# Queries on the state as four 64x64 tiles in two banks, with two weight pieces split by a summing transfer and the Nyquist row moved behind the mixing

## The reference, cut to what matters

```python
for t in range(S):
    state = alpha[:, :, t, :, None] * state + np.einsum('bhd,bhe->bhde', k[:, :, t], v[:, :, t])
    y[:, :, t] = np.einsum('bhd,bhde->bhe', q[:, :, t], state)
```

## Time and profile before

| | us |
|---|---|
| median of 3 runs | 721.84 |
| lowest, highest | 718.55, 721.86 |
| the profiled execution's own time | 720.12 |
| its span in the profile | 718.3 |

### The profile page before, as it was taken

The page is one execution under the profiler, slowest core; times in us unless marked ns, Lnnn a source line. Parts: engine busy times, 40 slices in busy tenths (PEclk is TensorE's granted clock), DMA queues, the critical chain, the costliest instruction groups (busy, mean ns, idle before and its releaser), DMA issues.

```text
span 718.3 us, 13452 instructions
## 1 busy us (share of the span) xinstructions
PE 701.0 (98%) x5578; PEld 670.6 (93%) x5578; DVE 451.8 (63%) x869; ACT 198.4 (28%) x369; POOL 80.0 (11%) x124
## 2 busy tenths in 40 slices
PE   7799989999999999999999999999999999999998
PEld 6689989889998999989999999999999999999998
DVE  7997868897768977668687747372543817331212
ACT  1438111242113411134415332232211422222111
POOL 1023000030001200042110512002210101000000
PEclk9999999999999999999999999999999999999999
DMA  9757132231332223061324403002110200000000
GB/s 295 208 139 182 52 100 84 83 97 55 91 93 71 63 54 97 35 212 44 112 77 165 144 20 92 1 34 67 53 59 1 76 23 33 0 34 1 5 29 34
DMA packets 21214, 55.90 MB, mean 78 GB/s; under 512 B 2388, under 2 KB 14808, under 8 KB 21160
## 3 DMA queue, kind: packets, MB, share of 16 engines
q1 hardware_dynamic: 18104, 44.53, 20.1%
q0 software_dynamic: 2912, 10.47, 5.6%
q10 hardware_dynamic: 144, 0.13, 0.1%
HBM read 45.66 MB, written 9.46 MB: 77 GB/s over the span
## 4 chain that ended last, share of the span: by engine, by line
PE 86%; DVE 10%; issue 2%; ACT 1%; DMA 1%; DVEq 0%; SPq 0%
PE bank L1178 74%; PE bank L1209 3%; PE bank L1241 2%; PE bank L1236 1%; PE bank L1273 1%; PE bank L1402 1%; PE bank L1388 1%; PE bank L1226 1%; DVE fwd L927 1%; DVE rev L915 1%; PE bank L1199 1%; DVE u_kept L1138 1%; DMA decay_k_q<-in_akq 1%; DVE sm L945 1%; DVE gated L1029 1%
## 5 line engine op out<-in xcount | busy, mean ns | idle before, releaser
L1178 PE MATMUL bank<-ut_hi,w_c 128*128 128x384 f32 x576 | 162.6, 338 | 0.0
L1125 DVE SCALAR_TENSOR_TENSOR hidden_lo<-bank,hidden_hi 128x384 fp32r<-128x384 f32 x96 | 53.3, 556 | 155.5 <-ACT hidden_hi L849 154.9
L1178 PEld LDWEIGHTS bank<-ut_hi,w_c 128*128 128x128 f32 x576 | 105.4, 188 | 0.4
L849 ACT ACTIVATE hidden_hi<-bank 128x384 fp32r<-128x384 f32 x96 | 47.2, 492 | 201.6 <-PE bank L1178 200.5
L1178 PE MATMUL bank<-w_c_hi,hidden_hi 128*128 128x384 f32 x288 | 96.6, 335 | 0.5 <-DVE u_kept L1138 0.5
L1178 PE MATMUL bank<-ut_lo,w_c 128*128 128x384 f32 x288 | 96.3, 334 | 0.0
L1178 PE MATMUL bank<-w_c_hi,hidden_lo 128*128 128x384 f32 x288 | 96.3, 334 | 0.0
L1178 PE MATMUL bank<-w_c_lo,hidden_hi 128*128 128x384 f32 x288 | 96.2, 334 | 0.0
L1178 PE MATMUL bank<-w_sg_hi,vn_hi 128*128 128x384 f32 x192 | 67.1, 350 | 0.0
L1178 PE MATMUL bank<-w_sg_lo,vn_hi 128*128 128x384 f32 x192 | 64.9, 338 | 0.0
L1178 PE MATMUL bank<-w_sg_hi,vn_lo 128*128 128x384 f32 x192 | 64.9, 338 | 0.0
(11 more groups left out here) (193 smaller groups left out, 1339.8 us busy)
## 6 DMA issues: line engine op xcount, KB each, us to landing
decay_k_q<-in_akq SPq DMA_DIRECT2D x19, 673.8 KB, 5.0
x_scratch<-x_half SPq DMA_DIRECT2D x8, 579.0 KB
out_tiles<-u_kept SPq DMA_DIRECT2D x24, 192.0 KB, 2.0
values<-in_v SPq DMA_DIRECT2D x18, 192.0 KB, 5.0
x_quarters<-x_scratch SPq DMA_DIRECT2D x16, 168.9 KB
raw_first_a<-in_w_first SPq DMA_DIRECT2D x3, 768.0 KB, 10.2
raw_first_b<-in_w_first SPq DMA_DIRECT2D x3, 768.0 KB
raw_weights_b<-in_w_second SPq DMA_DIRECT2D x3, 768.0 KB
```

The costliest lines, as they stand in the source:

```text
L849: nc.scalar.activation(hid[0][:, i % 4, :], HB[i % 2][:, 0:HS], ACT.Relu).then_inc(hhi_done, 1)
L1125: nc.vector.scalar_tensor_tensor(out=hid[1][:, i % 4, :], in0=HB[i % 2][:, 0:HS], scalar=0.0, in1=f32(hid[0][:, i % 4, :]), op0=ALU.max, o ...
L1178: ins = nc.tensor.matmul(dst, a, c, start=start and n == 0, stop=stop and n == len(passes) - 1)
```

## The change

In words:

1. **Queries on the state.** In step "out" all matmuls with values now come first, head by head, the first head of each pair to `ky` and the second to `sc[1]`, the bank with the second head's scores. The wait for `std_done` and the queries on the state come behind them, each head by itself: 48 rows, 64 columns of weights, 48 columns moving, in the order group, head, half. `y_done` rises by 4 for each chunk instead of 2, and all its waits are changed to match. ACT's copy gathers from the two banks.
2. **Pieces 6 and 7** of the weights join `SUMMED`. ACT's cast of piece 6 moves behind the four copies of z, that of piece 7 from step s 2 to behind the statistics of s 3; each is followed by the negative, and GpSimd issues the adding transfer there. DVE does nothing for them. The load of pieces 7 and 8 waits for the cast of the piece before instead of its subtraction.
3. **Nyquist** stands behind mix 0 on all engines, writes columns from 388 on of `FB[0]` and `FB[1]`, and waits for nothing of its own; ACT makes two copies instead of one. PE's wait for `ahr_done` goes; ACT waits for `ny_done` ahead of the copies of mix 1 and 2. GpSimd's step nyquist, and with it the gathering transfers of the quarters, moves behind its step mix 0, which waits for DVE's first statistics of that mixing.

The diff, cut to its core:

```diff
-SUMMED = (2, 3, 4)
+SUMMED = (2, 3, 4, 6, 7)
@@ P2_AT (P2_FIRST_AT in the same way)
-         10: [("nyquist", 0), ("mix", 0)], 11: [("stats", 0)],
+         10: [("mix", 0), ("nyquist", 0)], 11: [("stats", 0)],
@@ LAST_P1_AT
-              ("s", 1): [("split", 6), ("z", 0), ("z", 1), ("z", 2), ("z", 3)],
-              ("s", 2): [("nyquist", 0), ("split", 7), ("mix", 0), ("stats", 0)],
-              ("s", 3): [("mix", 1), ("stats", 1)], ("s", 4): [("mix", 2)],
+              ("s", 1): [("z", 0), ("z", 1), ("z", 2), ("z", 3), ("split hi", 6), ("neg", 6)],
+              ("s", 2): [("mix", 0), ("nyquist", 0), ("stats", 0)],
+              ("s", 3): [("mix", 1), ("stats", 1), ("split hi", 7), ("neg", 7)], ("s", 4): [("mix", 2)],
@@ GpSimd, phase1
+                            if what == "neg":
+                                sum_lo(n)
@@ ScalarE
-                nc.scalar.copy(yn[n % 2][:, c, :], ky[:, 0:DM]).then_inc(yn_done, 1)
+                nc.scalar.copy(yn[n % 2][:, c, :].rearrange("p (g j d) -> p j g d", j=2, d=D),
+                               banks[:, at - 1:at + 1, 0:G * D].rearrange("p j (g d) -> p j g d", g=G)[:, ::-1]
+                               ).then_inc(yn_done, 1)
...
-                    nc.scalar.copy(by_channel(fourier_tiles(m)[4][:]), by_parity(FB[1][0:1, 0:NL])).then_inc(ahr_done, 1)
+                    for odd in range(2):
+                        ins = nc.scalar.copy(by_channel(fourier_tiles(m)[4][:])[:, 0, odd], FB[odd][0:1, 2 * NL:2 * NL + KQ])
+                    ins.then_inc(ahr_done, 1)
                 if step == "mix":
                     act.wait_ge(mix_done, 2 * (KD * m + i + 1))
+                    if i > 0:
+                        act.wait_ge(ny_done, m + 1)
@@ TensorE, attend, step "out"
+                    y = [ky, sc[1]]
+                    for g in range(G):
+                        for j in range(2):
+                            cols = slice((2 * g + j) * D, (2 * g + j + 1) * D)
+                            for q in QUERIES:
+                                ins = nc.tensor.matmul(y[j][q, g * D:(g + 1) * D], sm[:, g, j, q], values[:, cols],
+                                                       start=g == 0, stop=c == 0, skip_group_check=True)
+                                if c == 0 and g == G - 1:
+                                    ins.then_inc(y_done, 1)
                     if c >= 1:
                         pe.wait_ge(std_done, (NT - 1) * n + c)
-                    for g in range(G):
-                        if c >= 1:
-                            for q in QUERIES:
-                                nc.tensor.matmul(ky[q, g * PP:(g + 1) * PP], qu[:, g, q], std[:, c % 2, g, :],
-                                                 start=True, stop=False, skip_group_check=True)
-                        ...
+                        for g in range(G):
+                            for j in range(2):
+                                at = slice(j * HR, j * HR + D)
+                                for q in QUERIES:
+                                    ins = nc.tensor.matmul(y[j][q, g * D:(g + 1) * D], qu[at, g, q],
+                                                           std[at, c % 2, g, j * D:(j + 1) * D], start=False, stop=True,
+                                                           skip_group_check=True)
+                                    if g == G - 1:
+                                        ins.then_inc(y_done, 1)
@@ TensorE, mixing and phase 2
-                    pe.wait_ge(z_kept, 4 * m + 2)
                     for odd in range(2):
-                        ins = nc.tensor.matmul(FB[1][0:2, odd * KQ:(odd + 1) * KQ], zz[0:KQ - odd, 0, odd, HS:HS + 2],
+                        ins = nc.tensor.matmul(FB[odd][0:2, 2 * NL:2 * NL + KQ], zz[0:KQ - odd, 0, odd, HS:HS + 2],
...
-                        if i == 2 and e == 0:
-                            pe.wait_ge(ahr_done, m + 1)
...
-                            wait_lo(pe, NP1 + KD - 2)
+                            for n in range(NP1, NP1 + KD - 1):
+                                wait_lo(pe, n)
```

More of the change, by code:

```diff
@@ L112 @@
          5: [("keep", 1), ("fold", 5), ("folded", 1)], 6: [("z", 0)], 7: [("z", 1)], 8: [("z", 2)], 9: [("z", 3)],
-         10: [("nyquist", 0), ("mix", 0)], 11: [("stats", 0)], 12: [("mix", 1)], 13: [("stats", 1)], 14: [("mix", 2)], 15: [("stats", 2)],
+         10: [("mix", 0), ("nyquist", 0)], 11: [("stats", 0)], 12: [("mix", 1)], 13: [("stats", 1)], 14: [("mix", 2)], 15: [("stats", 2)],
          16: [("norm", 0)], 17: [("turn", 0), ("norm", 1)], 18: [("turn", 1), ("turned", 0), ("norm", 2)],
@@ L118 @@
                6: [("fold", 0)], 7: [("fold", 1)], 8: [("fold", 2), ("fold", 4)], 9: [("fold", 3), ("folded", 0)],
-               10: [("fold", 5), ("folded", 1), ("z", 0)], 11: [("z", 1), ("z", 2)], 12: [("z", 3)], 13: [("nyquist", 0), ("mix", 0)],
+               10: [("fold", 5), ("folded", 1), ("z", 0)], 11: [("z", 1), ("z", 2)], 12: [("z", 3)], 13: [("mix", 0), ("nyquist", 0)],
                14: [("stats", 0)], 15: [("mix", 1)], 16: [("stats", 1), ("mix", 2)], 17: [("stats", 2)],
@@ L317, in build @@
                  place("raw_weights_c", [P, PIECE], F32, at_ug), place("raw_weights_d", [P, PIECE], F32, at_wo)]
-        bank = [ctx.enter_context(nc.psum_tensor(f"bank{i}", [P, 512], F32)) for i in range(8)]
+        banks = ctx.enter_context(nc.psum_tensor("banks", [P, 8, 512], F32))
+        bank = [banks[:, i, :] for i in range(8)]
         GB = bank[0:5]
-        SC, KY = bank[5:7], bank[7]
+        KY_AT = 7
+        SC, KY = bank[5:7], bank[KY_AT]
         HB, ACC, FB = bank[0:2], bank[2:5], bank[5:8]
@@ L446, in first_set, with first_at @@
         def first_set(c):
-            return (set_b, bank[2], bank[0:2]) if c % 2 else (set_a, KY, SC)
+            return (set_b, bank[first_at(c)], bank[0:2]) if c % 2 else (set_a, KY, SC)
+        def first_at(c):
+            return 2 if c % 2 else KY_AT
         def z_slot(i):
@@ L642, in v_scale, with sum_lo @@
                                         ALU.pow).then_inc(rs1_done, 1)
+            def sum_lo(n):
+                pool.wait_ge(w_neg_done, SUMMED.index(n) + 1)
+                src, m = (w_first, n) if n < NP1 else (w_second, n - NP1)
+                pool.dma_start(pieces[n][1], src[:, m * PIECE:(m + 1) * PIECE],
+                               accum_op=ALU.add).then_inc(w_sum_in[n], 16)
             def phase1(b):
@@ L731, in beside_last_phase1 @@
                         split_hi(n)
+                    elif what == "neg":
+                        negative(n)
                     elif what in FOURIER_STEPS:
@@ L865, in _ @@
                 elif step in ATTENTION_STEPS:
-                    attend(0, step, c, *first_set(c)[:2])
+                    attend(0, step, c, first_set(c)[0], first_at(c))
                 elif step == "u":
```

27 lines of the change are left out of this document (8 added, 19 removed).

## The result

The changed kernel took **724.01 us** (median of 7 runs, 722.67 to 725.39), the kernel before 720.26 beside it (7 runs, 718.55 to 721.86): ratio 1.0053, 95% interval 1.0039 to 1.0066. The forecast was 717.1 with a range up to 722.5. The profiled execution took 722.67, its span is 720.8.

A forecast was written before the change was run, and what follows sets the result against it. PE was taken to bound the kernel. Gains of 1.1, 1.4 and 1.0 us sum to 3.5, taken from the 720.6 average of four executions, giving 717.1 us; the range was about 714 to 722.5.

The forecast's parts named there:

- What bounds the kernel: Whole run: PE, busy 701.0 of 718.3 us, so only less PE work or less time between its instructions helps.
- the two long stretches: PE nearly always busy: 237.66 of 238.00 us from 102 to 340, and 318.57 of 320.00 from 380 to 700.
- Part 1: Queries on the state in step "out": block 1.53 instead of 1.60 us, 0.07 less for 16 chunks, 1.1 us gained.
- the two ends: Bounds of the gain from the queries on the state: -3.0 and +6.4 us around 1.1 gained.
- Part 2: Pieces 6 and 7, DVE's chain before 369 us: residual added at 356.0 instead of 357.68, 1.4 us gained.
- an end of 0: Lower end of the gain from pieces 6 and 7, if the transfer of the sum holds up the residual.
- The slip of SP's issues: Piece 7 and the residual issued 2.7 us later, at 350.4 and 351.1, as piece 7 waits for piece 6's cast.
- signs of being wrong: Queries at 0.7 or more, PE still waiting 1.4 us, a mixing pause without gathers, or a lost half clock window elsewhere.
- Part 3: Nyquist and gathers moved behind mix 0: pauses in two of four mixings, laid to GpSimd's gathers, vanish; 1.0 us gained.
- the first one: Weights gain nothing: residual lands at 357.7 or later, PE stands again at 369 us; 719.5 us, chance 0.2.
- The slower rival: Queries two at a time, row halves taking turns: block 2.00 us, each chunk loses 0.39; 724.5 us, chance 0.1.
- The floor for each record: Queries: each record costs at least 22.5 ns, block 1.79 us, each chunk loses 0.19; 721.2 us, chance 0.13.

The follow-up runs named there:

- part 1 alone: The kernel before with only the new order of the queries on the state (values first, four tiles, two banks); 719.20 us, ratio 1.0002.
- part1_two_tiles: The kernel before with only the new queries on the state, ordered row half outside, group inside; 722.09 us, ratio 1.0045.
- sum6_later: The changed kernel with the negative and adding transfer of piece 6 moved behind the statistics of mix 0; 719.47 us, ratio 1.0014.
- residual_first: The changed kernel with SP issuing the residual ahead of piece 7; 718.89 us, ratio 1.0004.

## Why the prediction was wrong, by its own steps

**What bounds the kernel: right.** PE bounds it; its busy time moved by 0.7 us. The loss came at the one place outside the two long stretches that the prediction had named, ahead of 369 us.

**Part 1: right in its working, too large in its count, too small to be measured.** Four tiles run at once. The forecast was 1.53 against 1.60, both without the 0.10 of leaving; with it the new block took 1.64 and the old one 1.70, so 0.06 less for 0.07. The count was 16 chunks. Those ahead of about 131 us don't count, since PE meets DVE there once more. PE's timeline at that point in three profiles, of the kernel before, of part 1 alone and of part1_two_tiles:

```profile
131.53 0.44 PE L1178 MATMUL bank<-w_out_hi,gated_hi 128*128 128x384 f32 x1 [0.34 <-DVE gated_lo L971]
```

```profile
131.43 0.45 PE L1192 MATMUL banks<-w_out_hi,gated_hi 128*128 128x384 f32 x1 [0.81 <-DVE gated_lo L985]
```

```profile
132.44 0.44 PE L1192 MATMUL banks<-w_out_hi,gated_hi 128*128 128x384 f32 x1 [0.19 <-DVE gated_lo L985]
```

In these three the faster PE is, the longer it waits: 0.19, 0.34 and 0.81. The five profiles with the old queries show 0.34 to 0.64 there, the eight with the new ones 0.53 to 1.07, so the two overlap, but on average 0.3 us goes back. Some 11 chunks are left, 0.6 to 0.7 us instead of 1.1. The run of part 1 alone, 1.0002 with an interval of 0.9986 to 1.0018, can't tell 0.6 from nothing; it excludes the two ends, 3.0 gained and 6.4 lost, and just about the 1.1.

**Part 2: the step that failed.** The prediction said "I put it at 356, the addition at 356.0 instead of 357.68". DVE was free as early as forecast (353.54; forecast some 354.5), and the wait for `x_half` went. But the residual was added at 361.68. Three errors lie in that step:

- It put the residual at 356 for a slip of SP's issues alone, and that was too early. sum6_later has this slip and no adding transfer: the residual is added 7.09 us behind the third gather, which by the clock of the kernel before (351.28) is 358.4, later than the 357.68 of DVE's own split. SP's last packet is in 6.6 us behind the third gather there, where it was 2.0 before: the slip of 2.6 us at the issue became 4.7 at the landing, with the packets now beside those of the gathers. GpSimd's gathers, half of the residual's rows, stand nowhere in the step. "Landed by 354.5 at the latest" was nearly right for the kernel before (last packet at 354.74, landed by the estimate above at 355.2), but it was carried over to a kernel in which more ran at the same time.
- It gave the adding transfer an end of 0 ("the transfer of the sum holds up the residual") and so said that it could cost nothing beyond the gain. The price of a late residual isn't bounded by what an early one brings. Here it was a pause of 4.6 us.
- It named SP's queue as what the issues pass through, and left out that the adding transfer shares the 16 DMA engines with the residual for 768 KB. "GpSimd gives two issues" is about the engine; the transfer behind the issue was costed at nothing. It took the addition from 7.09 us behind the third gather to 11.36.

The slip of SP's issues was put at 2.7 us. Against GpSimd's first gather it is 2.6 (piece 7 at 349.31 and the gather at 347.67, 1.64 behind it; before 347.67 and 348.64, 0.97 ahead). By the clock it was 1.3 to 1.6, since the changed profile reaches this stretch 1 us earlier, which is within the scatter of the two profiles of the kernel before.

A term that the sum lacked altogether is the half clock: the pause of 4.6 us cost 1.6 more, since PE's granted clock was 0.51 for 3.5 us behind it. The prediction named a half-clock window among its signs of being wrong, and priced it nowhere.

**Part 3: wrong.** "1.0 gained" rested on a coincidence in one profile, two mixings of four with a pause beside gathers. The control, the same kernel profiled again, has neither. What the move did bring, 0.5 us less wait for `x_half` by an earlier cast of piece 7, has no term in the sum; in the changed kernel piece 7 is no longer split there, so this has nothing to act on.

**The rivals.** The mechanism of the first one is what happened, the residual coming late, but its price stopped at a gain of nothing (719.5). The slower rival was put on the queries, where the trace had good rows, and not on the residual, where it had none; its time, 724.5, is near the measured one by chance. The floor for each record did not hold: 32 queries, with leaving, took 0.61 us, about 19 ns each. The Trainium skill (TensorE: Matmul & The Clock Gate, Back-to-back issue gap) states about 25 ns from start to start however small the matmul. By that they would take 0.80; the trace of this kernel disagrees, and the measurement decides.

## What to carry to other kernels

A transfer issued "in time" is not free: before moving a large one, list what small transfers are in flight behind it and who waits for them, on every queue and not on the one that is edited. Price a wait that might come by the work that depends on it, up to the next slack, not by the gain that it would cancel. And profile the unchanged kernel twice before reading a cause into a pause that only some of its repetitions show.

## What the runs showed of the hardware

- While an adding transfer (768 KB, fp32, from GpSimd's queue) ran, the DMA engines were 98.6% busy and moved 205 GB/s; with plain transfers, in packets mostly under 2 KB, they moved 396. Beside it a row of 1.5 KB on SP's queue took 11.47 us to land; without it, behind the same plain transfers, 7.2.
- Four tiles of 64 by 64 ran together: 32 fp32 matmuls of 48 columns in 0.61 us with leaving, against 0.88 with the same ones ordered so that most neighbours shared a row half.
- After a pause of PE of 4.6 us the granted clock was 0.51 for 3.5 us. The shorter pauses at the same place, in the kernel before, sum6_later and residual_first (1.4 to 1.8 us of waiting), were not followed by half clock: there the granted clock is 1.00 from 367 to 380 us.
- A short wait is no safe sign, though. Near 100 us PE of the kernel before waits 0.7 and then 1.5 us within 3 us, and this view of 102.90 to 106.30 us has it at half clock behind them, with products 0.32 us apart:

```profile
102.90:106.30 3.40, 3.40 (x13) 3.40 (x12) 1.29 (x2) 0.00 (x0) 0.00 (x0) 0.53 0.87 239
```
